# Block means of the first batch by products on TensorE, with a new order of the first jobs

## The chip, the cores and the metric

One core of a Trainium2 chip runs the whole program. The metric is the device time of one execution in microseconds; the median of three runs is used. The engines named below are PE (TensorE, matrix products), DVE (VectorE), ACT (ScalarE), POOL (GpSimd) and SP (SyncE, which here only issues DMAs).

## The reference

Attention over 2 batches of 8 heads, 768 tokens, head size 64: each query sees the keys within 15 tokens of it, and 24 summaries, one for each block of 32 tokens. The summary of the values is the block mean, `v_sum` below. Two MLPs with 512 to 2048 to 512 channels follow, over all 1536 tokens.

```python
k_sum = k.reshape(B, H, nb, block, D).max(axis=3)
v_sum = v.reshape(B, H, nb, block, D).mean(axis=3)
scores_l = scale * np.matmul(q, k.transpose(0, 1, 3, 2))
mask_l = np.abs(pos[:, None] - pos[None, :]) < window
scores_s = scale * np.einsum('bhsd,bhnd->bhsn', q, k_sum) + np.log(block)
a = softmax(concatenate([where(mask_l, scores_l, -1e9), scores_s]))   # in short
x = np.matmul(a, np.concatenate([v, v_sum], axis=2))                   # attention out
h = x @ w_in1;  x2 = (max(h, 0) + alpha * min(h, 0)) @ w_out1
h = x2 @ w_in2; out = (P(h) / (Q(h) + 1e-6)) @ w_out2                  # P cubic, Q quadratic
```

## The kernel before

**Jobs and stages.** The tokens are cut into four chunks of 384 (CH). An attention job is one pair of heads of one chunk: job j is pair j % 4 of chunk j // 4, 16 jobs in all. A job has the stages KQ (transposes of keys and queries on PE, copies by ACT, block maxima by DVE), KX (the rest of the keys, first chunk of a batch only), SC (scores on PE, mask and row minimum on DVE, exponential on ACT), NM (normalising on DVE), TR (transposes of the probabilities on PE, copied to `pt` by ACT) and PV (product with the values on PE, split into `x_hi` by ACT and `x_lo` by DVE). The value operand of a PV has 120 rows (KU): 96 rows of a window of values (KW) for each of six units of 64 queries, and below them the 24 block means, the same for each unit.

**The first chunk.** Jobs 0 to 3 run alone at the start, in orders written out by hand, one list an engine: FIRST_PE, FIRST_ACT, FIRST_DVE. WI and WO in FIRST_ACT are copies of a weight tile to `w_in_hi` or `w_out_hi`, each followed by a subtraction on POOL that makes the low part. RUN_UP puts products of the identity, read by nobody, ahead of a stage on PE, 26 in nine places. EARLY puts the first quarters of `hidden1(0)` and `hidden1(1)` between the last stages of jobs 2 and 3.

**The block means.** POOL makes them for four heads at once: `summarise_values(g)` adds 32 rows in a tree of five additions on 96 partitions, after a 768 KB load (`load_v_blocks`). For the first chunk `spread_first_sums` then writes them six times over into `vw0`, the values of jobs 0 to 3, by DMAs that POOL issues itself. `pt` is one buffer, so the copy of job j's probabilities waits for the PV of job j - 1 (`pe_v`).

**The loop of the first MLP.** STEPS = 64 steps, 16 a chunk. A step is `hidden1(i)` (12 products of 384 columns) and `output1(i - 2)` (12 more). Between them `slot(c + 1, f, n)` puts the stages of the next chunk's jobs, by the table SLOTS, and by SOON for the first job of the second chunk (job 4). `hidden1(i)` waits for `g1_low(i - 2)` on DVE, which waits for `g1_high(i - 2)` on ACT. In the first steps ACT also makes the high parts of the weights, in program order with everything else:

```python
if c == 0:
    for n in (f + 3,) if f < 2 else (2 * f + 1, 2 * f + 2) if f < 4 else (f + 5,):
        if n < FT:
            weights(0, n)
...
if i >= R1:
    act.wait_ge(pe_o, i - R1 + 1)
    g1_high(i)
```

so that tiles 5 and 6 come in step 2 ahead of `g1_high(2)`, and tiles 7 and 8 in step 3. Weight tiles are loaded by two: `load_w(0, 3)` brings tiles 6 and 7.

**The queue of loads.** SP issues all loads in one program order. `load_keys(5)` waits there for `pe_k` of job 4, that is, for the four key transposes of job 4 on PE, because both jobs use the same buffer. Behind it in the queue stand `load_values(4)` and `load_w(0, 3)`.

Of the kernel before, what the change touches and what calls it, by code (L numbers as in the profile page):

```python
# [13 lines left out]
def attention_two_mlps(nc, q, k, v, w_in1, w_out1, alpha, w_in2, w_out2, a_coef, b_coef, out):  # L14
# [32 lines left out]
    VG = 4  # L47
# [13 lines left out]
    KQ, KX, SC, NM, TR, PV, WI, WO = range(8)  # L61
# [5 lines left out]
    FIRST_PE = [(0, KQ), (0, KX), (1, KQ), (0, SC), (1, KX), (2, KQ), (0, TR), (1, SC), (2, KX), (3, KQ),  # L67
                (1, TR), (2, SC), (3, KX), (3, SC), (0, PV), (2, TR), (1, PV), (3, TR), (2, PV), (4, KQ), (3, PV)]

    FIRST_ACT = [(0, KQ), (1, KQ), (0, SC), (2, KQ), (0, TR), (1, SC), (3, KQ), (1, TR), (2, SC), (0, PV),  # L70
                 (3, SC), (0, WI), (2, TR), (1, PV), (1, WI), (3, TR), (2, PV), (4, KQ), (3, PV), (0, WO), (2, WI), (1, WO),
                 (2, WO)]

    FIRST_DVE = [(0, KQ), (0, KX), (1, KQ), (0, SC), (1, KX), (0, NM), (2, KQ), (1, SC), (2, KX), (1, NM), (3, KQ),
                 (2, SC), (3, KX), (2, NM), (3, SC), (0, PV), (3, NM), (1, PV), (2, PV), (4, KQ), (3, PV)]
# [24 lines left out]
    vs_raw1 = place("vs_raw1", [P, BLOCK * D], offset=w_end - (UNITS * H + BLOCK) * D * 4)  # L100
# [12 lines left out]
    vs_raw0 = place("vs_raw0", [P, BLOCK * D], offset=top)  # L113
# [6 lines left out]
    vs_raw = [vs_raw1 if g == 1 else vs_raw0 for g in range(VG)]  # L120
# [4 lines left out]
    kx_raw = place("kx_raw", [P, 4, 2, D])  # L125
    q_raw = place("q_raw", [P, QTILES, 2, D])
# [6 lines left out]
    pt = place("pt", [P, UNITS, P])  # L133
# [3 lines left out]
    g_neg = place("g_neg", [P, CH])  # L137
    g1_hi = place("g1_hi", [P, R1, CH], F32R)
# [15 lines left out]
    with ExitStack() as ctx:  # L154
# [19 lines left out]
        sums0_loaded = [sem(f"sums0_loaded{n}") for n in range(2)]  # L174
# [8 lines left out]
        pe_s, pe_t, pe_v = sem("pe_s"), sem("pe_t"), sem("pe_v")  # L183
# [26 lines left out]
        def batch(j):  # L210
            return chunk(j) // 2
# [11 lines left out]

        def kx_jobs(j):

            return sum(1 for n in range(j + 1) if half(n) == 0)
# [16 lines left out]
        def vgroup(j):  # L243
            return batch(j) * 2 + pair(j) // 2
# [12 lines left out]
        def _(sp):  # L257
# [5 lines left out]
            def load_first_keys(p):  # L263
                hs = heads(p)
                load_pair(k_raw0[:, :, hs, :], KROWS[0], k[0, hs, 0:4 * KROWS[0], :], k0_loaded[p])
                load_pair(q_raw0[:, :, hs, :], P, q[0, hs, 0:CH, :], q0_loaded[p])
                load_pair(kx_raw0[:, :, hs, :], KXROWS, k[0, hs, 4 * KROWS[0]:S, :], kx0_loaded[p])
# [30 lines left out]
            def load_first_edges():  # L298
# [4 lines left out]
            def load_first_windows(p):  # L303
                for h in range(2 * p, 2 * p + 2):
                    sp.dma_start(vw0[0:KW, 1:UNITS, h, :], windows_of(0, h, 0)).then_inc(v0_loaded[p], 16)

            def load_values(j):
                b, h0, s = batch(j), 2 * pair(j), j % 2
                if j >= NPAIR + 2:
                    sp.wait_ge(pe_v, j - 1)  # L310
                t0, t1 = (1, UNITS) if half(j) == 0 else (0, UNITS - 1)
                for h in range(2):
                    sp.dma_start(vw[0:KW, s, t0:t1, h, :], windows_of(b, h0 + h, half(j))).then_inc(v_loaded[s], 16)
                t, rows, inside, outside = edge(half(j))
                sp.dma_start(vw[rows, s, t, :, :], v[b, h0:h0 + 2, inside, :].rearrange("h p d -> p h d")).then_inc(v_loaded[s], 16)
                sp.dma_start(vw[outside, s, t, :, :], v[b, h0:h0 + 2, 0:WINDOW, :].rearrange("h p d -> p h d")).then_inc(v_loaded[s], 16)
                sp.wait_ge(pool_vs, vgroup(j) + 1)
                for h in range(2):
                    r = (pair(j) % 2) * 2 * NB + h * NB
                    src = vsum[r:r + NB, vgroup(j), :].unsqueeze(1).broadcast_to([NB, UNITS, D])  # L320
                    sp.dma_start(vw[KW:KU, s, :, h, :], src).then_inc(v_loaded[s], 16)

            def load_v_blocks(g):
                if g >= 2:
                    sp.wait_ge(pool_vs, 2 * g - 3)
                sp.dma_start(vs_raw[g][0:4 * NB, :],
                             v[g // 2, 4 * (g % 2):4 * (g % 2) + 4].rearrange("h (n j) d -> (h n) (j d)", j=BLOCK)).then_inc(vs_loaded[g], 16)
# [26 lines left out]
            load_first_edges()  # L354
            load_first_windows(0)
            load_first_windows(1)
# [4 lines left out]
            load_w_out(0, 0)  # L361
            load_w(0, 1)
# [12 lines left out]
            load_v_blocks(2)  # L375
            load_values(6)
            load_keys(7)
            load_v_blocks(3)
# [16 lines left out]
        def _(pool):  # L395
# [23 lines left out]

            tree = 0  # L420

            def summarise_values(g):

                nonlocal tree
                pool.wait_ge(vs_loaded[g], 16)
                n = BLOCK * D // 2
                while n >= D:
                    rows = vs_raw[g][0:4 * NB]
# [4 lines left out]
                pool.tensor_scalar(vsum[0:4 * NB, g, :], vs_raw[g][0:4 * NB, 0:D], 1.0 / BLOCK, 1.0,  # L433
                                   ALU.mult, ALU.mult).then_inc(pool_vs, 1)

            def spread_first_sums(g):

                pool.wait_ge(pool_vs, g + 1)
                for h in range(4):
                    pool.dma_start(vw0[KW:KU, :, 4 * g + h, :],  # L440
                                   vsum[h * NB:(h + 1) * NB, g, :].unsqueeze(1).broadcast_to([NB, UNITS, D])).then_inc(sums0_loaded[g], 16)
# [12 lines left out]
            for g in range(2):  # L454
                summarise_values(g)
                spread_first_sums(g)
            for f in range(WG):
                split_w_in(f)
            for f in range(FT):
                if f >= WG:  # L460
                    split_w_in(f)
                split_w_out(0, f)
                if f in (11, 15):
                    summarise_values(2 + f // 15)
# [16 lines left out]
        def _(act):  # L481
# [3 lines left out]
            def attention(j, stage):  # L485
# [30 lines left out]
                elif stage == TR:  # L516
                    for h in range(2):
                        act.wait_ge(pe_t, 2 * j + h + 1)
                        if j and h == 0:
                            act.wait_ge(pe_v, j)  # L520
                        copy(pt[0:KU, h * UP:(h + 1) * UP, :].rearrange("p n c -> p (n c)"), bk[h][0:KU, 0:UP * P]).then_inc(act_pt, 1)
# [13 lines left out]

# [266 lines left out]
        def _(pe):  # L802
            def attention(j, stage):
# [12 lines left out]
                if stage == KQ:  # L816
# [8 lines left out]
                    if first:  # L825
                        pe.wait_ge(q0_loaded[p], 32)
                    else:
# [20 lines left out]
                elif stage == TR:  # L848
                    for g in range(2):
# [3 lines left out]
                        last.then_inc(pe_t, 1)  # L853
                elif stage == PV:
                    if first:
                        pe.wait_ge(edges0_loaded, 32)
                        pe.wait_ge(v0_loaded[p], 32)
                        pe.wait_ge(sums0_loaded[p // 2], 16 * 4)
# [3 lines left out]
                    for u in range(UNITS):  # L862
                        for h in range(2):
                            rows, tokens = slice(h * QT, (h + 1) * QT), slice((u % 2) * QT, (u % 2 + 1) * QT)
                            values = vw0[0:KU, u, 2 * p + h, :] if first else vw[0:KU, s, u, h, :]
                            last = pe.matmul(bk[0][rows, u * QT:(u + 1) * QT], values, pt[0:KU, h * UP + u // 2, tokens],  # L866
# [91 lines left out]

            pe.wait_ge(pool_ready, 1)
            for j, stage in FIRST_PE:  # L960
                spare = acc[3] if FIRST_PE.index((j, stage)) < FIRST_PE.index((3, KQ)) else att[1]
                for _ in range(RUN_UP.get((j, stage), 0)):
                    pe.matmul(spare[:, 0:P], ident[:, :], ident[:, :], start=True, stop=True)
                attention(j, stage)
                for i, pairs in EARLY.get((j, stage), []):
                    hidden1(i, pairs)
# [3 lines left out]
            for i in range(STEPS):  # L970
                c, f = i // FT, i % FT
                begun = [kk for parts in EARLY.values() for n, pairs in parts for kk in pairs if n == i]
                hidden1(i, range(len(begun), KD))
# [43 lines left out]
```

## Time and profile before

| what | value |
|---|---|
| median of 3 runs | 632.59 us (632.51 to 634.97) |
| profiled execution, its own time | 633.66 us |
| its span, first to last instruction | 631.8 us |
| PE busy | 613.3 us, 97% of the span |
| weight loads into PE | 571.4 us, 90% |
| DVE, ACT, POOL busy | 413.6, 309.0, 201.5 us |
| PE in the chain that ended last | 92% |
| bytes moved by DMA | 37.60 MB |

A busy share is a mean over stages of different kinds. The share of a stretch, and what ends the idle time in it, is read from the windows, the timelines and the chain. All times are microseconds from the start of the span.

### The profile page before, as it was taken

Reading aid. Unit: us, or ns where it says so; the run is one execution under the profiler, and the core shown is the slowest. Engines: PE = TensorE matmul, PEld = TensorE weight load, DVE = VectorE, ACT = ScalarE, POOL = GpSimd, SP = SyncE. Lnnn points to the kernel's source line nnn. Section 1 sums busy time; section 2 is a strip of 40 time slices with the busy share of each in tenths; the row PEclk is TensorE's granted clock in tenths of the full one; section 3 lists DMA queues with packets and bytes.
Section 4 is the critical chain, followed back from the end, with each engine's and each line's share of the span. In section 5 each row is a group of like instructions: output and inputs, shape, how many; then the busy total and the mean of one; then the engine's idle time right before and its main releaser. Section 6 shows DMA issues by size and latency. Waiting matters only on the chain.

```text
span 631.8 us, 10645 instructions
## 1 busy us (share of the span) xinstructions
PE 613.3 (97%) x3941; PEld 571.4 (90%) x3941; DVE 413.6 (65%) x953; ACT 309.0 (49%) x774; POOL 201.5 (32%) x224
## 2 busy tenths in 40 slices
PE   7588999999999999999999999999999999999998
PEld 7478999999999999999999989899989998999996
DVE  4445554566456544555555499878887888788775
ACT  4267544342232423232234477656765666556654
POOL 2839676000000000000133366334443444334431
PEclk9688999999999999999999999999999999999999
DMA  8978862022201221001433300001000000001001
GB/s 181 211 201 240 220 124 49 14 63 61 57 15 42 50 50 40 11 2 34 125 110 106 127 34 1 1 0 52 1 0 2 23 29 1 0 2 51 0 2 50
DMA packets 79187, 37.60 MB, mean 60 GB/s; under 512 B 56624, under 2 KB 73024, under 8 KB 78752
## 3 DMA queue, kind: packets, MB, share of 16 engines
q1 hardware_dynamic: 78880, 36.63, 22.8%
q8 instruction: 31, 0.51, 0.3%
q0 software_dynamic: 256, 0.30, 0.2%
q14 instruction: 20, 0.16, 0.1%
HBM read 32.58 MB, written 3.15 MB: 57 GB/s over the span
## 4 chain that ended last, share of the span: by engine, by line
PE 92%; DVE 2%; DMA 2%; SPq 1%; POOL 1%; ACT 1%; issue 0%; ACTq 0%; DVEq 0%; POOLq 0%
PE acc L876 15%; PE acc L878 14%; PE acc L877 14%; PE hid L876 11%; PE hid L878 10%; PE hid L877 10%; PE att L876 4%; PE att L878 4%; PE att L877 4%; PE att L866 2%; PE att L812 2%; PE att L845 1%; SPq L261 1%; PE att L852 1%; DMA vs_raw<-in_v_dram 1%; POOL vs_raw L429 1%
## 5 line engine op out<-in xcount | busy, mean ns | idle before, releaser
L876 PE MATMUL hid<-x_hi,w_in_hi 128*128 128x384 f32 x384 | 130.9, 341 | 2.6 <-DVE g_lo L725 1.8
L878 PE MATMUL hid<-x_hi,w_in_lo 128*128 128x384 f32 x384 | 129.8, 338 | 0.0
L877 PE MATMUL hid<-x_lo,w_in_hi 128*128 128x384 f32 x384 | 129.5, 337 | 0.0
L451 POOL TENSOR_TENSOR w_out_lo<-w_out_raw,w_out_hi 128x512 fp32r<-128x512 f32 x32 | 41.3, 1292 | 239.8 <-ACT w_out_hi L483 239.8
L876 PE MATMUL acc<-g_hi,w_out_hi 128*128 128x384 f32 x256 | 91.2, 356 | 0.0
L473 POOL TENSOR_SCALAR qpart<-habs,ab 128x384 f32<-128x384 f32 x64 | 44.0, 688 | 143.1 <-ACT poly L627 142.4
L878 PE MATMUL acc<-g_hi,w_out_lo 128*128 128x384 f32 x256 | 86.8, 339 | 0.0
L877 PE MATMUL acc<-g_lo,w_out_hi 128*128 128x384 f32 x256 | 86.5, 338 | 0.0
L483 ACT ACTIVATE g_hi<-hid 128x384 fp32r<-128x384 f32 x96 | 48.4, 504 | 71.1 <-PE acc L878 63.7
L725 DVE TENSOR_TENSOR g_lo<-hid,g_hi 128x384 fp32r<-128x384 f32 x64 | 35.6, 556 | 66.3 <-ACT g_hi L483 66.3
L876 PEld LDWEIGHTS hid<-x_hi,w_in_hi 128*128 128x128 f32 x384 | 72.5, 189 | 4.9 <-POOL w_in_lo L446 2.1
L878 PE MATMUL acc<-w_out_hi,g_lo 128*128 128x512 f32 x192 | 76.1, 396 | 0.0
L877 PE MATMUL acc<-w_out_lo,g_hi 128*128 128x512 f32 x192 | 75.6, 394 | 0.0
L876 PE MATMUL acc<-w_out_hi,g_hi 128*128 128x512 f32 x192 | 75.5, 393 | 0.0
L877 PEld LDWEIGHTS hid<-x_lo,w_in_hi 128*128 128x128 f32 x384 | 72.6, 189 | 1.3
L878 PEld LDWEIGHTS hid<-x_hi,w_in_lo 128*128 128x128 f32 x384 | 72.5, 189 | 0.0
L748 DVE TENSOR_SCALAR g_neg<-hid,prelu_alpha 128x384 f32<-128x384 f32 x64 | 39.4, 616 | 48.9 <-PE hid L878 48.9
L475 POOL TENSOR_TENSOR qpart<-qpart,habs 128x384 f32<-128x384 f32 x64 | 65.7, 1026 | 5.3
L876 PEld LDWEIGHTS acc<-g_hi,w_out_hi 128*128 128x128 f32 x256 | 48.2, 188 | 2.6 <-issue 1.7
L877 PEld LDWEIGHTS acc<-g_lo,w_out_hi 128*128 128x128 f32 x256 | 48.3, 189 | 0.0
L878 PEld LDWEIGHTS acc<-g_hi,w_out_lo 128*128 128x128 f32 x256 | 48.1, 188 | 0.0
L513 ACT ACTIVATE att<-att,nmax 128x120 f32<-128x120 f32 x78 | 24.7, 368 | 44.4 <-DVE nmax L693 44.4
(145 smaller groups left out, 1159.6 us busy)
## 6 DMA issues: line engine op xcount, KB each, us to landing
w_in_raw<-in_moe_w_in_dram SPq DMA_DIRECT2D x32, 256.0 KB, 4.2
w_out_raw<-in_moe_w_out_dram SPq DMA_DIRECT2D x16, 512.0 KB, 4.2
vw<-in_v_dram SPq DMA_DIRECT2D x32, 120.0 KB, 5.3
q_raw<-in_q_dram SPq DMA_DIRECT2D x32, 96.0 KB, 2.6
vs_raw<-in_v_dram SPq DMA_DIRECT2D x4, 768.0 KB, 7.0
out_dram<-out_sb SPq DMA_DIRECT2D x12, 256.0 KB, 2.0
k_raw<-in_k_dram SPq DMA_DIRECT2D x16, 104.0 KB
k_raw<-in_k_dram SPq DMA_DIRECT2D x16, 100.0 KB
```

Source lines behind the costliest of these rows:

```text
L451: pool.tensor_tensor(w_out_lo[:, f, :], w_out_raw[:, f, :], w_out_hi[f][:, :].bitcast(F32), ALU.subtract).then_inc(pool_w_out, 1)
L473: pool.tensor_scalar(qpart[:, i % 2, :], habs[:, i % 2, :], ab[:, 5:6], ab[:, 4:5], ALU.mult, ALU.add).then_inc(pool_qb, 1)
L475: pool.tensor_tensor(qpart[:, i % 2, :], qpart[:, i % 2, :], habs[:, i % 2, :], ALU.mult).then_inc(pool_q, 1)
L483: return act.activation(dst, src, ACT.Identity)
L513: last = act.activation(scores_of(bk, h, n), scores_of(bk, h, n), ACT.Exp, scale=-1.0, bias=nmax[:, s, i:i + 1], accum_out=sums_of(bk, h)[ ...
L725: dve.tensor_tensor(g1_lo[:, i % R1, :], hid[i % 2][:, 0:CH], g1_hi[:, i % R1, :].bitcast(F32), ALU.subtract).then_inc(dve_g, 1)
L748: dve.tensor_scalar(g_neg[:, :], hb, 0.0, prelu_alpha[:, f:f + 1], ALU.min, ALU.mult).then_inc(dve_m, 1)
L812: tr = pe.transpose(dst[:, t * rows:(t + 1) * rows], rows_of_pair.rearrange("p h d -> p (h d)"), ident[0:rows, 0:rows])
L866: last = pe.matmul(bk[0][rows, u * QT:(u + 1) * QT], values, pt[0:KU, h * UP + u // 2, tokens], start=True, stop=True)
L876: pe.matmul(dst, lhs[0], rhs[0], start=start, stop=False)
L877: pe.matmul(dst, lhs[0], rhs[1], start=False, stop=False)
L878: return pe.matmul(dst, lhs[1], rhs[0], start=False, stop=stop)
```

## The change

The block means of batch 0 are made on PE: a stage AV of ten accumulating products for each job multiplies six windows of values, and four tiles of the rest of the sequence (`v_rest`), by shifted columns of a matrix `avg` that holds 1/32 at the rows of a block. The means of a pair arrive in rows 96 to 119 of a PSUM bank, where ACT (stage SU) copies them six times over into `vw0`. POOL's tree stays for batch 1; a copy on POOL keeps the means of batch 0 for chunk 1 (`keep_first_sums`). `pt` has two buffers. The three lists are new; the early quarters of `hidden1` stand in FIRST_PE as HD, all eight; job 4's KQ moves from the lists to the loop (step 0), its SC to step 2. Weight subtractions on POOL run in another order. The first loads are issued in another order. The identity's products are 19 in five places.

```diff
-    SOON = {(0, 1): [SC], (1, 1): [NM], (2, 1): [TR], (3, 0): [PV]}
+    SOON = {(0, 2): [KQ], (2, 0): [SC], (2, 2): [NM], (3, 0): [TR], (3, 2): [PV]}
+    FIRST_PE = [(0, KQ), (0, KX), (1, KQ), (0, SC), (1, KX), (2, KQ), (1, SC), (0, AV), (0, TR), (2, KX), (3, KQ),
+                (2, SC), (1, AV), (1, TR), (3, KX), (0, PV), (2, AV), (3, SC), (2, TR), (3, AV), (1, PV), (2, PV),
+                (3, TR), (0, HD), (3, PV), (0, HD), (0, HD), (1, HD), (0, HD), (1, HD), (1, HD), (1, HD)]
+    RUN_UP = {(0, KQ): 8, (0, KX): 3, (0, SC): 3, (1, SC): 2, (2, KX): 3}
+    FIRST_ACT = [(0, KQ), (1, KQ), (0, SC), (2, KQ), (0, SU), (0, TR), (1, SC), (3, KQ), (1, SU), (1, TR), (2, SC),
+                 (2, SU), (0, PV), (2, TR), (3, SC), (0, WI), (1, PV), (3, SU), (3, TR), (1, WI), (2, PV), (3, PV),
+                 (2, WI), (0, WO), (1, WO), (2, WO)]
-    RUN_UP = {(0, KQ): 8, (0, KX): 2, (1, KQ): 1, (0, SC): 2, (0, TR): 4, (2, TR): 3, (1, PV): 2, (3, TR): 2, (2, PV): 2}
-    EARLY = {(3, TR): [(0, (0, 1))], (2, PV): [(1, (0, 1))], (3, PV): [(0, (2,)), (1, (2,))]}
...
-    pt = place("pt", [P, UNITS, P])
+    pt = place("pt", [P, 2, UNITS, P])
...
+            def first_rest(p):
+                hs = heads(p)
+                sp.dma_start(v_rest[0:RP, hs, :], v[0, hs, CH:S, :].rearrange("h (p t) d -> p h (t d)", t=RT)).then_inc(rest0_loaded[p], 16)
...
-            load_first_keys(0)
-            load_first_keys(1)
-            load_first_keys(2)
-            load_v_blocks(0)
-            load_first_keys(3)
-            load_v_blocks(1)
+            first_k(0)
+            first_q(0)
+            first_kx(0)
+            first_k(1)
+            first_q(1)
+            first_kx(1)
+            first_rest(0)
+            first_k(2)
+            first_q(2)
+            first_edges()
+            first_windows(0)
+            first_k(3)
+            first_q(3)
+            first_kx(2)
+            first_rest(1)
+            first_windows(1)
+            first_kx(3)
+            first_windows(2)
+            first_rest(2)
...
             load_w_in(0, 0)
-            load_first_windows(2)
-            load_first_windows(3)
-            load_keys(4)
+            first_windows(3)
+            first_rest(3)
             load_w_out(0, 0)
-            load_w(0, 1)
+            load_w_in(0, 1)
+            load_keys(4)
+            load_w_out(0, 1)
...
+            own = avg[0:KW, KW + 2 * (UNITS - 1):KW + 2 * UNITS]
+            own_rest = avg[0:RP, AW + KW + CH // BLOCK:AW + KU]
+            pool.memset(avg[:, :], 0.0).then_inc(pool_avg, 1)
...
+            def keep_first_sums():
+
+                pool.wait_ge(act_su, NPAIR)
+                pool.wait_ge(pool_w_in, WG)
+                pool.tensor_copy(vsum0.rearrange("p a h d -> p (a h d)"),
+                                 vw0[KW:KU, 0, :, :].rearrange("p h d -> p (h d)")).then_inc(pool_v0, 1)
+                pool.wait_ge(pool_v0, 1)
...
-            for g in range(2):
-                summarise_values(g)
-                spread_first_sums(g)
-            for f in range(WG):
-                split_w_in(f)
+            split_w_in(0)
+            split_w_in(1)
+            keep_first_sums()
+            split_w_in(2)
             for f in range(FT):
-                if f >= WG:
-                    split_w_in(f)
                 split_w_out(0, f)
+                if f + 3 < FT:
+                    split_w_in(f + 3)
...
-                        if j and h == 0:
-                            act.wait_ge(pe_v, j)
+                        if j >= 2 and h == 0:
+                            act.wait_ge(pe_v, j - 1)
...
+                elif stage == SU:
+                    act.wait_ge(pe_av, j + 1)
+                    copy(vw0[KW:KU, :, heads(p), :].rearrange("p u h d -> p u (h d)"),
+                         means_of(j)[KW:KU, :].unsqueeze(1).broadcast_to([NB, UNITS, P])).then_inc(act_su, 1)
...
+                elif stage == AV:
+                    if j == 0:
+                        pe.wait_ge(pool_avg, 5)
+                        pe.wait_ge(edges0_loaded, 32)
+                    pe.wait_ge(v0_loaded[p], 32)
+                    pe.wait_ge(rest0_loaded[p], 16)
+                    if j == 1:
+                        pe.wait_ge(act_pt, 2)
+                    if j:
+                        pe.wait_ge(act_su, j)
+                    means = means_of(j)[0:KU, :]
+                    for u in range(UNITS):
+                        at = 2 * (UNITS - 1 - u)
+                        pe.matmul(means, avg[0:KW, at:at + KU], vw0[0:KW, u, heads(p), :].rearrange("p h d -> p (h d)"),
+                                  start=u == 0, stop=False)
+                    for t in range(RT):
+                        last = pe.matmul(means, avg[0:RP, AW:AW + KU], v_rest[0:RP, heads(p), t * D:(t + 1) * D],
+                                         start=False, stop=t == RT - 1)
```

## Rows read from the trace of the kernel before

**Rows 1.** Windows: us, busy us and count per engine, PEclk, DMA share, GB/s.

```profile
16.00:29.30 13.30, 6.49 (x76) 4.47 (x70) 6.73 (x37) 2.96 (x15) 12.32 (x14) 0.68 1.14 217
...
62.70:631.80 569.10, 564.60 (x3496) 529.69 (x3495) 383.76 (x829) 275.85 (x663) 163.90 (x175) 1.00 0.16 43
```

**Rows 2.** Chain that ended last: start us, us, what.

```profile
9.63 6.24 DMA vs_raw<-in_v_dram
...
24.08 4.96 DMA vw<-vsum
...
29.32 1.57 PE att L866 x24
```

**Rows 3.** Timeline of POOL: start, us, line, op, tiles, count [idle <-releaser].

```profile
1.20 0.29 POOL L398 TENSOR_SCALAR_AFFINE_SELECT ident<-ident 128x128 f32<-128x128 f32 x1 [0.25 <-POOL ident L396]
...
16.02 5.42 POOL L429 TENSOR_TENSOR vs_raw<-vs_raw 96x1024 f32<-96x1024 f32 x5 [10.22 <-DMA vs_raw<-in_v_dram]
...
38.03 1.27 POOL L446 TENSOR_TENSOR w_in_lo<-w_in_raw,w_in_hi 128x512 fp32r<-128x512 f32 x1 [4.85 <-ACT w_in_hi L483]
```

**Rows 4.** Timeline of PE, same columns.

```profile
12.22 1.06 PE L963 MATMUL acc<-ident 128*128 128x128 f32 x8
...
38.40 0.82 PE L852 MATMUL acc<-ident,probs 128*120 128x128 f32 x6
...
41.64 0.92 PE L866 MATMUL acc<-pt,vw 120*64 120x64 f32 x24
42.49 0.44 PE L876 MATMUL hid<-x_hi,w_in_hi 128*128 128x384 f32 x1
...
43.12 0.33 PE L876 MATMUL hid<-x_hi,w_in_hi 128*128 128x384 f32 x1
...
43.89 0.56 PE L812 MATMUL att<-ident,k_raw 100*128 100x100 f32 x4
...
44.72 0.92 PE L866 MATMUL acc<-pt,vw 120*64 120x64 f32 x24
...
47.54 0.85 PE L845 MATMUL att<-kt,qt 64*64 64x120 f32 x24
...
50.94 0.41 PE L876 MATMUL hid<-x_hi,w_in_hi 128*128 128x384 f32 x1 [1.84 <-DVE g_lo L725]
...
62.70 0.34 PE L876 MATMUL hid<-x_hi,w_in_hi 128*128 128x384 f32 x1
...
64.81 0.51 PE L812 MATMUL att<-ident,k_raw 100*128 100x100 f32 x4
```

**Rows 5.** Windows of two us, columns as in the first group.

```profile
20.00:22.00 2.00, 1.70 (x28) 1.41 (x27) 0.76 (x2) 0.01 (x1) 1.52 (x4) 0.67 1.21 174
36.00:38.00 2.00, 2.00 (x28) 1.69 (x27) 1.86 (x9) 1.95 (x11) 0.00 (x0) 0.56 1.06 257
52.00:54.00 2.00, 2.00 (x8) 2.00 (x7) 1.88 (x6) 2.00 (x5) 1.72 (x2) 0.50 0.85 250
```

**Rows 6.** Timeline of SP's DMA issues.

```profile
44.49 0.79 SPq L261 DMA_DIRECT2D k_raw<-in_k_dram  x2
...
51.01 1.07 SPq L334 DMA_DIRECT2D w_in_raw<-in_moe_w_in_dram  x2
52.13 0.51 SPq L341 DMA_DIRECT2D w_out_raw<-in_moe_w_out_dram  x1
```

**Rows 7.** DMA issues at 18.4, 51.0, 52.1 us: KB each, us to landing.

```profile
vw<-in_v_dram SPq DMA_DIRECT2D x2, 120.0 KB, 5.7
...
w_in_raw<-in_moe_w_in_dram SPq DMA_DIRECT2D x2, 256.0 KB, 3.1
...
w_out_raw<-in_moe_w_out_dram SPq DMA_DIRECT2D x1, 512.0 KB, 5.5
```

**Rows 8.** Timeline of ACT.

```profile
56.26 0.88 ACT L483 ACTIVATE pt<-att 120x384 f32<-120x384 f32 x2 [2.12 <-PE att L852]
...
58.58 0.63 ACT L483 ACTIVATE w_out_hi<-w_out_raw 128x512 fp32r<-128x512 f32 x1
```

More of the change, by code:

```diff
@@ L46, in attention_two_mlps @@
     QTILES = CH // P
-    VG = 4
+    VG = 2
+    RT = 4
+    RP = (S - CH) // RT
     STEPS = NCH * FT
@@ L112, in attention_two_mlps @@
     x_lo = place("x_lo", [P, 2, KD, CH], F32R)
-    vs_raw0 = place("vs_raw0", [P, BLOCK * D], offset=top)
+    vs_raw = place("vs_raw", [P, BLOCK * D], offset=top)
+    v_rest = place("v_rest", [P, H, RT * D], offset=top)
     y_raw = place("y_raw", [P, 2, KD, CH])
@@ L137, in attention_two_mlps @@
     g_neg = place("g_neg", [P, CH])
+    AW = KU + 2 * (UNITS - 1)
+    avg = place("avg", [P, AW + KU], offset=top - CH * 4)
     g1_hi = place("g1_hi", [P, R1, CH], F32R)
@@ L173, in attention_two_mlps @@
         edges0_loaded = sem("edges0_loaded")
-        sums0_loaded = [sem(f"sums0_loaded{n}") for n in range(2)]
+        rest0_loaded = [sem(f"rest0_loaded{p}") for p in range(NPAIR)]
         k_loaded, kx_loaded, q_loaded = sem("k_loaded"), sem("kx_loaded"), sem("q_loaded")
@@ L243, in vgroup @@
         def vgroup(j):
-            return batch(j) * 2 + pair(j) // 2
+            return pair(j) // 2
         def banks(j):
@@ L427, in summarise_values @@
                 while n >= D:
-                    rows = vs_raw[g][0:4 * NB]
+                    rows = vs_raw[0:4 * NB]
                     pool.tensor_tensor(rows[:, 0:n], rows[:, 0:n], rows[:, n:2 * n], ALU.add).then_inc(pool_tree, 1)
@@ L432, in summarise_values @@
                     n //= 2
-                pool.tensor_scalar(vsum[0:4 * NB, g, :], vs_raw[g][0:4 * NB, 0:D], 1.0 / BLOCK, 1.0,
+                pool.tensor_scalar(vsum[0:4 * NB, g, :], vs_raw[0:4 * NB, 0:D], 1.0 / BLOCK, 1.0,
                                    ALU.mult, ALU.mult).then_inc(pool_vs, 1)
[L436 to L441, printed above, removed]
+            def keep_first_sums():
[4 more added lines that the diff above has]
+                pool.wait_ge(pool_v0, 1)
             def split_w_in(f):
@@ L534, in w_in_high @@
                 act.wait_ge(w_in_loaded[f // WG], 16 * WG * (m + 1))
+                if m == 0 and f == 3:
+                    act.wait_ge(pool_v0, 1)
                 copy(w_in_hi[f][:, :, :].rearrange("p k c -> p (k c)"), w_in_raw[:, f, :, :].rearrange("p k c -> p (k c)")).then_inc(act_w_in, 1)
@@ L865, in attention @@
                             values = vw0[0:KU, u, 2 * p + h, :] if first else vw[0:KU, s, u, h, :]
-                            last = pe.matmul(bk[0][rows, u * QT:(u + 1) * QT], values, pt[0:KU, h * UP + u // 2, tokens],
+                            last = pe.matmul(bk[0][rows, u * QT:(u + 1) * QT], values, pt[0:KU, s, h * UP + u // 2, tokens],
                                              start=True, stop=True)
@@ L957, in output2 @@
                         mm.then_inc(pe_y, 1)
+            begun = [0, 0]
             pe.wait_ge(pool_ready, 1)
             for j, stage in FIRST_PE:
-                spare = acc[3] if FIRST_PE.index((j, stage)) < FIRST_PE.index((3, KQ)) else att[1]
                 for _ in range(RUN_UP.get((j, stage), 0)):
[L963 to L966, printed above, removed]
+                    pe.matmul(acc[2][:, 0:P], ident[:, :], ident[:, :], start=True, stop=True)
+                if stage == HD:
+                    hidden1(j, [begun[j]])
+                    begun[j] += 1
+                else:
+                    attention(j, stage)
                 if (j, stage) == (2, PV):
@@ L971, in _ @@
                 c, f = i // FT, i % FT
-                begun = [kk for parts in EARLY.values() for n, pairs in parts for kk in pairs if n == i]
-                hidden1(i, range(len(begun), KD))
+                if i >= 2:
+                    hidden1(i)
                 slot(c + 1, f, 0)
```

76 lines of the change are left out of this document (48 added, 28 removed).

## The prediction

> **What bounds the kernel now.** I read the windows of the whole span first, to see where PE is not busy. From 62.7 us to the end it works 564.6 of 569.1 us at full granted clock [rows 1]. No instruction of that stretch is taken away, so there is nothing to win there, and the page's 97% for PE says the same. What is open lies before 62.7. From 16.0 to 29.3 PE works 6.49 of 13.30 us [rows 1]. The chain that ended last says why: a 768 KB load of value blocks (6.24 us from 9.63), POOL's tree, the DMA of the means into the values (4.96 us from 24.08), and only then the first PV at 29.32 [rows 2]. POOL's own timeline adds that it sat idle for 10.22 us before the tree, and that the five additions took 5.42 us [rows 3]. In this thin stretch the granted clock fell (mean 0.67 in 20 to 22 us) and it was still at its lower level, 1.2 GHz, for most of 36 to 38 us (mean 0.56) [rows 5]. So the beginning is bound by one chain through DMA and POOL. A second place is at 50.94, where PE waited 1.84 us for `g_lo` [rows 4] and the clock fell again (0.50 in 52 to 54) [rows 5].
>
> **The place where both kernels are compared.** I compare the start of `hidden1(4)`, at 62.70 before [rows 4]. By then both programs have done the same products of the MLP (steps 0 to 3, outputs 0 and 1) and all of job 4. Behind it the order on PE is the same, so whatever this point gains is the gain of the run, if no later stall is new.
>
> **Part 1: the block means leave the chain.** AV needs the windows of values, `v_rest` and `avg`. The two fills and four selects that make `avg` are bounded below by nothing and above by 0.29 us each, the select over 128 columns [rows 3]: under 2 us, on a POOL that is idle until 16.02 [rows 3]. Cost: nothing, and about 1 us if POOL were late. The values of pair 0 are in the queue behind 2176 KB in all (two pairs of keys and queries with their rest 1152, `v_rest` 192, k2 and q2 400, edges 192, windows 240). At 217 GB/s, that is 212 KB a us [rows 1], it takes 10.3 us, and with the first issue at 0.75 us and some 3 us until a queue that is still being filled is in full flow I take 14.8 us as the landing (13.5 to 17.0: the late end is an issue at 11.3 plus the 5.7 us that a window took to land [rows 7]). So the first AV starts at about 14.8, where the old chain gave 29.3 to the first PV.
>
> **Part 2: what PE does from there.** It is now the engine with the longest queue. Four products of the identity, 8 instructions, take 1.06 us with a last one of 0.25, so one instruction is 0.115 us [rows 4]. An AV is ten such products, 20 instructions: 2.3 us. No row shows these; the bounds are 0.09 and 0.18 us an instruction (1.8 to 3.6 us for an AV), the upper one if weights of 120 shifted columns cannot be loaded beside the products. I take 2.3 since the products of the identity have the same shape. In the order of FIRST_PE, from the start of the first AV to the end of job 4's key transposes:
> - four AV: 9.2 us;
> - four TR at 0.60 (six transposes, 0.82 busy with 0.2 of tail): 2.4;
> - three products of the identity: 0.7;
> - two KX at 0.40 and KQ of job 3 at 0.83 (43.89 to 44.72): 1.6;
> - two SC at 0.78 (0.85 busy): 1.6;
> - four PV at 0.85 (41.64 to 42.49): 3.4;
> - eight quarters of `hidden1` at 0.60 (0.63 from 42.49 to 43.12): 4.8;
> - the transpose of alpha 0.2, and four key transposes 0.5.
> All from [rows 4]; the sum is 24.4. ACT and DVE have less: ACT 4.9 us for each job (KQ 1.1, exponentials 1.8, SU 0.8, `pt` 0.9, `x_hi` 0.4), DVE some 5. SU is a copy of 768 columns; `pt` takes 0.44 for 384 and a weight tile of 512 columns 0.52 to its successor [rows 8], so 0.8, bounds 0.5 and 1.1. In my order of the stages on the three engines PE then waits only some tenths for `x_lo` and for a scale of the probabilities; I add 0.4. Job 4's key transposes end at 14.8 + 24.4 + 0.4 = 39.6 us, before at 44.45 (43.89 and 0.56) [rows 4]. That is 4.85 us earlier. The second buffer of `pt` is what lets TR run ahead of PV; its cost is nothing. The copy of the means on POOL (bounds 0.3 and 1.3, the subtraction of 512 columns [rows 3]) stands ahead of the third weight subtraction, which is done at about 38.3 and needed at 40: hidden; uncovered it would cost up to 1.3.
>
> **Part 3: what comes late next.** KQ of job 4 now stands directly ahead of `hidden1(2)`, where it was 50.94 - 44.72 = 6.2 us ahead [rows 4]. SP waits for it before it issues anything more: the keys of job 5 went out at 44.49, `w_in` 6 and 7 at 51.01 and `w_out` 6 and 7 at 52.13 [rows 6]. The latter landed 5.5 us later, at 57.6 [rows 7]. The same queue, moved by 4.85, lands it at 52.8. ACT wants it in step 2, ahead of `g1_high(2)`, at about 46.5, and it is in program order: `g1_high(2)`, both copies of job 4's `pt` and everything after them stand behind the wait. Copy of tile 6 0.5, `g_hi` 0.4, two `pt` 0.88 [rows 8], PV of job 4 0.85 [rows 4]: `hidden1(4)` starts at 52.8 + 2.65 = 55.45. PE alone would be there sooner: from 40.0 it has two `hidden1` and two `output1` of 2.11 (62.70 to 64.81 [rows 4]), SC 0.78, TR 0.6 and PV 0.85, to 50.7. So PE stands still for 4.8 us. Before, an idle time of 1.84 was enough to bring the clock down soon after; I expect that here too. PV at the low clock is 1.57 [rows 2] instead of 0.92 [rows 4]: 0.65; and the products that follow cost up to twice for a while. For both I take 1.8, bounds 0 and 3: the low stretch before was about 3.5 us long, which at half rate loses 1.75. `hidden1(4)` counts as started at 57.2, so the gain is 62.7 - 57.2 = 5.5 us.
>
> **Part 4: what costs nothing.** Seven products of the identity fewer: they stood in idle time. The loads: 1536 KB of blocks go, 768 KB of `v_rest` come, and 288 KB of means on POOL's queue go, so the first weight tiles come earlier (I have `w_in` 0 at about 25, wanted at 31). POOL's new order of subtractions puts the tree of batch 1 about three steps of ACT later; its means are wanted a chunk later. If that cover were gone, a wait of up to 5.4 us (the tree [rows 3]) could stand at the change of chunk.
>
> **The sum.** Span 631.8 - 5.5 = 626.3. The profiled execution took 633.66, 1.86 more than its span and 1.07 above the median of 632.59; against its own time the sum gives 628.2, against the median 627.1. I forecast 627.1. Its own range is 624.5 to 629.5 (AV 1.8 to 3.6 us each is the widest term, and then the clock).
>
> **Rivals.**
> - *Weights are no wait.* If ACT is not held up by tiles 6 and 7, `hidden1(4)` starts at 50.7 to 51.0 and the gain is 11.7: 620.9. Against it: SP's seven microseconds of issues ahead of those tiles [rows 6] are the same ones. For it: fewer bytes are in flight then. 10%.
> - *The first values come late.* If windows land at 17.0 rather than 14.8, PE idles over 3 us after the second SC, with a stretch of transposes before it. 2.2 us are lost, and the clock may fall, which costs another 2: a gain of 1.3, 631.3. For it: window DMAs took 5.7 us [rows 7] and they stand behind ten other issues. 18%.
> - *Slower: the clock stays low through the first jobs.* Before, it was low for some 16 us, from about 21 to 38 [rows 5], with short blocks and waits between them. If it falls ahead of the first AV and does not come back until the quarters of `hidden1`, each block costs about 1.75 times as much (PV 1.57 for 0.92). Over 20 us of low clock that loses 20 x (1 - 1/1.75) = 8.6 us, and the result is 635.7. It decides against the change from about 13 us of low clock. Against it: AV is 2.3 us of dense products, four times, with hardly a gap. 8%.
> - *The means are not what held PV.* Then the first PV would still come at 29; but the chain of waits names the DMA of the means directly. Near 632.6; 4%.
>
> On the third rival the Trainium skill speaks against this change. "TensorE: Matmul & The Clock Gate", section "HAM oscillation — how this bites in real kernels", says that bursts of products with waits for data between them each begin at half clock. By that rule every AV that waits for its values would run at 1.2 GHz, four times 2.3 more, and the sum would be some 9 us later, an estimate. The trace agrees for the wait at 50.94, and for the thin stretch from 16 us on.
>
> **How the numbers follow.** Forecast 60%, the rivals 10, 18, 8 and 4%. The range has to leave out no more than 2 in 10: it takes the forecast's own range, the late values (to 632) and the larger part of the first rival: 621.5 to 632.0. About 0.5%, 3.2 us, is what a measurement can tell from no change, so faster means below 629.4. The forecast lies there nearly whole (57 of 60), the first rival too, and of the late values a third: 0.73. Slower than 635.8: 0.07. Within: 0.20.
>
> **What would show it.** The first AV at 14 to 15.5 us and 2.3 us long; no DMA from `vsum` and no tree on POOL in the first 60 us; key transposes of job 4 near 39 us; then a wait of 3 to 6 us on PE before PV of job 4 or `hidden1(4)`, ended by ACT's `pt` or `g_lo`, with ACT idle until a copy of `w_out_raw`; a low clock behind it; `hidden1(4)` at 55 to 57; from there the same 569 us. The prediction is wrong if AV takes 3.6 us, if the clock is low between 15 and 38 us, or if the tiles 6 and 7 land before ACT wants them.

## The result and the profile after

The changed kernel takes 627.15 us, the median of four runs (626.75 to 628.32), against 633.04 for the kernel before: ratio 0.990, interval 0.9881 to 0.9918. On another chip later it was 628.00 against 634.53, 0.9902 (0.9883 to 0.9921). The forecast was 627.1. The span of the profiled execution went from 631.8 to 626.6 us; that execution of the changed kernel, at 628.32 us, is the slowest of its four, so spans show 5.2 us of gain where the medians show 5.9.

The windows of the changed kernel, columns as in [rows 1]:

```profile
16.00:29.30 13.30, 12.60 (x163) 11.54 (x162) 8.62 (x44) 9.81 (x37) 0.00 (x0) 1.00 0.97 235
...
62.70:626.60 563.90, 559.39 (x3464) 524.52 (x3462) 382.45 (x825) 272.52 (x656) 160.97 (x172) 1.00 0.16 42
```

From 16 to 29.3 us PE is busy for 12.60 us where it was 6.49, and the granted clock is full where its mean was 0.68 [rows 1]. POOL, with 12.32 us of tree and DMA issues in that stretch before, does nothing there. Behind 62.7 us nothing was won.

The timeline of PE in the changed kernel (start, us, line, op, out<-in, count, and in brackets the idle time before and what ended it):

```profile
11.76 0.58 PE L869 MATMUL acc<-ident,k_raw 104*128 104x104 f32 x4 [1.50 <-DMA k_raw<-in_k_dram]
...
13.88 0.85 PE L904 MATMUL hid<-kt,qt 64*64 64x120 f32 x24
14.88 1.54 PE L926 MATMUL acc<-vw,avg 96*120 96x128 f32 x12
...
17.13 0.82 PE L911 MATMUL att<-ident,probs 128*120 128x128 f32 x6
...
29.56 1.54 PE L926 MATMUL att<-vw,avg 96*120 96x128 f32 x12 [0.51 <-issue]
...
39.89 0.51 PE L869 MATMUL att<-ident,k_raw 100*128 100x100 f32 x4
...
41.08 0.41 PE L954 MATMUL hid<-x_hi,w_in_hi 128*128 128x384 f32 x1 [0.35 <-DVE g_lo L782]
...
51.03 0.33 PE L956 MATMUL acc<-g_hi,w_out_lo 128*128 128x384 f32 x1
55.07 1.11 PE L944 MATMUL att<-pt,vw 120*64 120x64 f32 x24 [3.71 <-ACT pt L535]
56.12 0.69 PE L954 MATMUL hid<-x_hi,w_in_hi 128*128 128x384 f32 x1
...
59.64 0.51 PE L869 MATMUL att<-ident,k_raw 100*128 100x100 f32 x4
```

The first AV starts at 14.88 and takes 2.25 us (to 17.13). Job 4's key transposes end at 40.40 (39.89 and 0.51), before at 44.45 [rows 4]. Then the new wait: PE is through with `output1(1)` at 51.4 and stands still for 3.71 us until ACT has copied the probabilities of job 4 to `pt`. The keys of job 5, which come directly behind `hidden1(4)`, start at 59.64, before at 64.81 [rows 4]. That is 5.17 us earlier, and the span is 5.2 us shorter: all of the gain is made by this point. What stands behind the wait is shown by the queues of SP and ACT:

```profile
40.43 0.79 SPq L269 DMA_DIRECT2D k_raw<-in_k_dram  x2
...
47.26 0.51 SPq L365 DMA_DIRECT2D w_out_raw<-in_moe_w_out_dram  x1
```

```profile
50.05 0.63 ACT L535 ACTIVATE w_in_hi<-w_in_raw 128x512 fp32r<-128x512 f32 x1 [1.59 <-DMA w_in_raw<-in_moe_w_in_dram]
53.16 0.63 ACT L535 ACTIVATE w_out_hi<-w_out_raw 128x512 fp32r<-128x512 f32 x1 [2.48 <-DMA w_out_raw<-in_moe_w_out_dram]
...
54.07 0.86 ACT L535 ACTIVATE pt<-att 120x384 f32<-120x384 f32 x2
```

SP issues nothing from 32.4 us to 40.43, when job 4's key transposes are done, and comes to `w_out` of tiles 6 and 7 at 47.26. ACT waits 1.59 us for `w_in` and 2.48 us for `w_out` of tile 6, and `g_hi` and both copies of `pt` come after them. The chain of the changed kernel that ended last goes the same way:

```profile
47.26 5.88 DMA w_out_raw<-in_moe_w_out_dram
...
55.07 1.11 PE att L944 x24
```

The clock fell behind that wait, not in it. Windows of two us, with PEclk third from the end:

```profile
52.00:54.00 2.00, 0.00 (x0) 0.00 (x0) 0.00 (x0) 0.84 (x2) 1.25 (x2) 1.00 1.08 325
54.00:56.00 2.00, 0.93 (x24) 0.95 (x24) 1.65 (x3) 0.93 (x3) 0.00 (x0) 0.91 1.07 351
56.00:58.00 2.00, 2.00 (x10) 1.89 (x7) 0.56 (x1) 1.78 (x4) 0.69 (x1) 0.50 1.13 324
58.00:60.00 2.00, 2.00 (x13) 1.96 (x12) 0.72 (x2) 1.17 (x3) 2.00 (x3) 0.74 0.99 180
```

The mean of 0.91 comes from its end: the clock is still full from 55.2 to 55.6, half a microsecond into the PV, and at its lower level, 1.2 GHz, right after. So more than half of the PV ran at the full clock (1.11 us, between the 0.92 and 1.55 of a PV at either level) and most of `hidden1(4)` at the lower one.

### The profile page after: what moved, and what is told of

The parts are those of the page before. It is cut to its first block, busy times and chain, and to the rows that moved or that the text cites. A ratio compares the mean times of both kernels' runs of the same rounds, so it can differ in the third digit from the quotient of the medians.

```text
span 626.6 us, 10782 instructions
## 1 busy us (share of the span) xinstructions
PE 612.4 (98%) x4007; PEld 573.3 (92%) x4007; DVE 415.6 (66%) x953; ACT 311.8 (50%) x778; POOL 187.6 (30%) x212
## 4 chain that ended last, share of the span: by engine, by line
PE 93%; SPq 2%; DMA 2%; DVE 1%; ACT 1%; issue 1%; ACTq 0%
PE acc L954 15%; PE acc L956 14%; PE acc L955 14%; PE hid L954 10%; PE hid L955 10%; PE hid L956 10%; PE att L954 4%; PE att L956 4%; PE att L955 4%; PE att L944 2%; PE att L869 1%; PE att L904 1%; SPq L269 1%; PE att L911 1%; DMA w_out_raw<-in_moe_w_out_dram 1%; PE att L926 1%
```

## The experiments

Eleven variants were run, and the changed kernel once more. Each ratio is to the kernel before on the same chip, with its 95% interval. The changed kernel stands at 0.9901 (mean of its two). 0.001 is 0.63 us.

### The wait for weights: two ways round it

Edit of `w3_ahead`:

```diff
             load_w(0, 2)
+            load_w(0, 3)
             load_keys(5)
             load_values(4)
-            load_w(0, 3)
```

> The changed kernel with the loads of weight tiles 6 and 7 issued ahead of the keys of job 5, so that they no longer stand behind the wait for job 4's key transposes. Theory (in the changed kernel ACT's copies of job 4's probabilities stand behind the copy of w_out tile 6, which lands 12.8 us after those transposes): PE's wait of 3.7 us before the PV of job 4 goes, the granted clock stays at its upper level, hidden1(4) is as fast as its neighbours; what is left is up to 1 us of waiting for the values of job 4, which are issued 1.6 us later. 4.3 to 5.3 us below the changed kernel's 627.15, so 622 to 623. Rival (the wait has another cause that comes at nearly the same time, such as the values of job 4 or POOL's subtractions): under 1.5 us gained, 625.7 or more.

Measured: 622.33 us, 0.9813 (0.9795 to 0.9831): 5.6 us below the changed kernel. Its PE timeline:

```profile
38.23 0.51 PE L869 MATMUL att<-ident,k_raw 100*128 100x100 f32 x4
...
49.63 0.92 PE L944 MATMUL att<-pt,vw 120*64 120x64 f32 x24
...
52.69 0.51 PE L869 MATMUL att<-ident,k_raw 100*128 100x100 f32 x4
```

PV of job 4 has no wait. From job 4's keys to job 5's it is 14.46 us (52.69 less 38.23), in the changed kernel 19.75 (59.64 less 39.89). So 5.3 us are the price of the stall with its low clock, and the values of job 4, issued later, were still in time. The clock stays full to the end (mean 1.0). Its profiled execution is 6.9 us shorter than the changed kernel's, more than the 5.6 us of the ratios, because its first loads also happened to land earlier: the first AV starts at 13.98, 0.9 us before the changed kernel's, and job 4's keys at 38.23, 1.7 us before.

Edit of `tile6_later`, on ACT, with the loads untouched:

```diff
-                    for n in (f + 3,) if f < 2 else (2 * f + 1, 2 * f + 2) if f < 4 else (f + 5,):
+                    for n in (f + 3,) if f < 3 else (6, 7, 8) if f == 3 else (f + 5,):
```

> The changed kernel with the copies of weight tile 6 moved on ACT from step 2 to step 3, behind g1_high(2) and the probabilities of job 4; the loads are as they were. If the order on ACT passes the late load on to PE, PV of job 4 starts at about 51.5 us without a wait, and only g1_high(3) is late: a stall of 0 to 1.5 us at hidden1(5). 3.5 to 5.3 us below 627.15. If the late tiles are needed by PE itself at that time, or ACT is late for another reason, nothing is gained (626.5 to 627.5).

Measured: 623.31 us, 0.9826 (0.9806 to 0.9846), 4.8 us below the changed kernel. The timeline of ACT:

```profile
48.09 0.87 ACT L535 ACTIVATE pt<-att 120x384 f32<-120x384 f32 x2
...
54.78 0.63 ACT L535 ACTIVATE w_out_hi<-w_out_raw 128x512 fp32r<-128x512 f32 x1 [0.30 <-DMA w_out_raw<-in_moe_w_out_dram]
```

`pt` is copied at 48.09, six us earlier than in the changed kernel, and no wait appears on PE. The loads are as late as they were, so it was the order on ACT that handed a late load to PE; the tiles themselves were not needed yet. Either change removes the stall, and the two agree.

### What held the first jobs before: means and buffer

Three versions of the kernel before. `before_pt2` has the second buffer of `pt`, with `act.wait_ge(pe_v, j - 1)` for j of 2 and more, and nothing else. `before_no_means` leaves out the block means of the first chunk and puts zeros in their rows. With them go POOL's four DMAs for each group of heads (288 KB in all) and the wait for them; the trees on POOL stay:

```diff
+            pool.memset(vw0[KW:KU, :, :, :], 0.0).then_inc(sums0_loaded[0], 1)
             tree = 0
...
-                spread_first_sums(g)
...
-                        pe.wait_ge(sums0_loaded[p // 2], 16 * 4)
+                        pe.wait_ge(sums0_loaded[0], 1)
```

> The kernel before with two buffers of transposed probabilities and nothing else of the change. Theory (the means' chain is the wall and the single buffer only passes it on): the probabilities of jobs 1 to 3 are ready before the means arrive, the PVs of jobs 0 and 1 follow at 29 to 31 us, and PV of job 2 waits for the second set of means at about 38 us, before 41.6: 2 to 3.5 us faster than before. Rival (the single buffer is the larger half of the loss): 5 us or more. Rival (the buffer is not on the path): under 0.5.

Measured: 630.99 us, 0.9951 (0.9935 to 0.9968), 3.1 us faster.

> The kernel before with the block means of the first chunk left out (zeros in their rows; the trees on POOL stay for the second chunk, the DMAs that spread them and the wait for them go). One buffer of probabilities as before. Theory: the first PV starts when the windows of pair 0 have landed and the scores of job 3 are done, at about 25 instead of 29.3 us, and everything behind it moves with it: 3 to 4.5 us faster than before. If something else bounds the first PV: under 1 us.

Measured: 630.64 us, 0.9939 (0.9916 to 0.9961), 3.9 us faster by the ratio.

> The kernel before with both: two buffers of probabilities and no block means in the first chunk. Theory: means and buffer together are the whole wall, so this gains more than the two alone together, 6 to 11 us against before, limited by the landing of windows (31 us) and weights; the step list then meets the wait for weight tiles 6 and 7. If the two gains only add up: 5 to 7 us.

Measured: 625.62 us, 0.9872 (0.9850 to 0.9894), 8.1 us faster. The same places in the three timelines of PE, the first PV and job 4's keys:

```profile
30.99 1.55 PE L866 MATMUL att<-pt,vw 120*64 120x64 f32 x24 [5.60 <-DMA vw<-vsum]
...
39.81 0.92 PE L866 MATMUL acc<-pt,vw 120*64 120x64 f32 x24
...
42.06 0.56 PE L812 MATMUL att<-ident,k_raw 100*128 100x100 f32 x4
```

```profile
26.56 1.55 PE L866 MATMUL att<-pt,vw 120*64 120x64 f32 x24 [1.42 <-issue]
...
41.15 0.56 PE L812 MATMUL att<-ident,k_raw 100*128 100x100 f32 x4
```

```profile
26.20 1.55 PE L866 MATMUL att<-pt,vw 120*64 120x64 f32 x24
...
36.43 0.56 PE L812 MATMUL att<-ident,k_raw 100*128 100x100 f32 x4
...
43.48 0.41 PE L876 MATMUL hid<-x_hi,w_in_hi 128*128 128x384 f32 x1 [1.84 <-DVE g_lo L725]
```

With the buffer alone PE waits 5.60 us for the DMA of the means, and PV of job 2 comes at 39.81, before at 41.64 [rows 4]. With the means alone gone the first PV comes at 26.56, before at 29.32 [rows 2], but the next copies of `pt` still queue behind the PVs, as ACT's timeline of that run shows:

```profile
28.21 0.87 ACT L483 ACTIVATE pt<-hid 120x384 f32<-120x384 f32 x2 [8.66 <-PE att L866]
```

Together job 4's keys start at 36.43: 7.5 us earlier than before, against 1.8 and 2.7 for each alone. In these executions the two are worth more together than apart, though part of that is chance: the execution of `before_pt2` is the slowest of its six, and its first PV, at 30.99, came 1.7 us later than before. From job 4's keys to job 5's it is 20.9 us in the kernel before and with either change alone, and 20.0 with both, where the clock stayed up. The times do not settle it: 1.28% for both against 1.10% for the sum, which is inside the intervals. That each of the two is on the path, and that both together are worth 8.1 us, is shown.

### The buffer in the new order

`after_pt1` is the changed kernel with the old rule for `pt`: slot 0 always, and a wait for the PV before.

> The changed kernel with one buffer of transposed probabilities, and each copy of them waiting for the PV before, as in the kernel before; all else as changed. Theory: ACT's copies for jobs 1 to 3 wait for the PVs of jobs 0 to 2, and with them the exponentials of jobs 2 and 3; job 4's key transposes end 3 to 4 us later and so does everything: 2.5 to 4.5 us slower than 627.15, around 630.5. If the second buffer is not needed in this order: within 1 us of 627.15.

Measured: 634.00 us, 1.0002 (0.9986 to 1.0017). The whole gain is gone, 6.4 us and not 2.5 to 4.5. The two timelines, ACT and PE:

```profile
33.31 0.87 ACT L535 ACTIVATE pt<-acc 120x384 f32<-120x384 f32 x2 [3.37 <-PE hid L944]
```

```profile
43.48 0.51 PE L869 MATMUL att<-ident,k_raw 100*128 100x100 f32 x4
...
59.62 1.55 PE L944 MATMUL att<-pt,vw 120*64 120x64 f32 x24 [4.65 <-ACT pt L535]
...
64.98 0.51 PE L869 MATMUL att<-ident,k_raw 100*128 100x100 f32 x4
```

The mechanism is the expected one: ACT stands 3.37 us for a PV, and job 4's keys come at 43.48, 3.6 us later. What was mis-sized is what follows: the wait on PE behind it is 4.65 instead of 3.71 us, the PV runs wholly at the low clock (1.55 us), and job 5's keys are 5.3 us later than in the changed kernel (64.98 against 59.64). So the buffer is no detail: in this order it is worth as much as the whole change.

### How much of the start is PE's own work

`short_av` leaves out the four products with `v_rest` in each AV (the means of the later blocks of batch 0 are then missing).

> The changed kernel with the four products of the rest of the sequence left out of each AV (the block means of the later part of batch 0 are then wrong): 8 instructions of about 0.11 us less, four times, 3.6 us of PE's work between 15 and 33 us. If PE alone bounds the first jobs, as the prediction's sum took it: 3.2 to 3.6 us faster than 627.15. If ACT, DVE and the loads stand close behind PE: 1 to 2 us faster. If the loads bound it: under 0.5.

Measured: 624.71 us, 0.9864 (0.9825 to 0.9903); three of its four runs lie between 624.46 and 624.73. By the ratio it is 2.3 us faster than the changed kernel at 0.9901, which its interval just includes, and by the medians 3.4. In its profile job 4's keys start at 36.65, 3.2 us earlier, of which 0.7 came with an earlier first AV (14.16). That leaves 2.5 of the 3.6 us removed. One row of its PE timeline, and the landing of `v_rest` of pair 3, issued at 21.87, show where 0.9 of the rest went:

```profile
27.22 1.54 PE L926 MATMUL att<-vw,avg 96*120 96x128 f32 x12 [0.89 <-issue]
```

```profile
v_rest<-in_v_dram SPq DMA_DIRECT2D x1, 192.0 KB, 5.3
```

21.87 and 5.3 us give 27.2, where the last AV starts. The answer lies between the two expectations: in this profile PE bounds most of the stretch, and the loads, rather than ACT or DVE, stand about 1 us behind it.

### The products of the identity

`few_run_up` keeps only the first eight: `RUN_UP = {(0, KQ): 8}`.

> The changed kernel without the products of the identity but the first eight: 11 of 19 are left out. If they only fill time: 0.4 to 1.0 us faster than 627.15 (three of them stand on the path after the first AV, 0.65 us, the others in waits for loads). If they hold the clock: the granted clock falls before or in the first AV, the AVs of jobs 0 and 1 take up to 4.5 us instead of 2.3, and the run is 2 to 5 us slower than 627.15.

Measured: 628.01 us, 0.9895 (0.9878 to 0.9912), no difference from the changed kernel. But the profile is not the same:

```profile
13.99 2.88 PE L926 MATMUL acc<-vw,avg 96*120 96x128 f32 x12 [0.44 <-DMA vw<-in_v_dram]
...
18.37 1.49 PE L911 MATMUL att<-ident,probs 128*120 128x128 f32 x6
...
40.65 0.51 PE L869 MATMUL att<-ident,k_raw 100*128 100x100 f32 x4
...
54.87 1.55 PE L944 MATMUL att<-pt,vw 120*64 120x64 f32 x24 [2.75 <-ACT pt L535]
```

The clock was at 0.50 from 14 to 20 us, the first AV took 4.38 us (13.99 to 18.37) instead of 2.25, and still job 4's keys were only 0.8 us later. The longer AV, the transposes behind it and the next keys cost 3.1 us. Against that, this execution's first AV had started 0.9 us earlier, the three products on the path (0.67 us) were gone, and behind the scores of job 2 another 0.8 us went, the pause at 29.56 among it; the other eight products had stood in waits. Then PE's wait for the weights came out at 2.75 instead of 3.71 us and took the rest in, although the whole PV behind it ran at the low clock. So I took the stall away and tried again. `w3_few_run_up` and `w3_no_kx2` both have the loads of `w3_ahead`; the second drops only the three products ahead of job 2's KX.

> The loads of tiles 6 and 7 ahead, as in w3_ahead, and only the first eight products of the identity. In few_run_up the clock was at 1.2 GHz from 13.9 to 20.3 us and the step list was 0.8 us late at job 4's keys, while the wait for weights behind it was 1 us shorter. Without that wait nothing can give the time back. If the eleven products pay for themselves by the clock: 0.5 to 1.5 us slower than w3_ahead (0.9813 of before), 0.982 to 0.984. If not: equal or faster.

> The loads of tiles 6 and 7 ahead, as in w3_ahead, and the three products of the identity ahead of job 2's KX left out (16 stay). They stand behind ten dense products of an AV and ahead of transposes, a score stage and the next AV. If the clock holds without them: 0.3 to 0.7 us faster than w3_ahead, 0.980 to 0.981 of before. If it falls between 18 and 20 us: 1 to 2 us slower than w3_ahead.

Measured on one chip: 624.46 us, 0.9841 (0.9821 to 0.9862), runs from 623.01 to 624.78, and 621.78 us, 0.9802 (0.9784 to 0.9820), runs from 621.08 to 622.11. The eight products by which they differ are worth 2.7 us once nothing behind hides it. Against `w3_ahead`, on another chip, all eleven are worth 1.8 us by the ratios, a little over the expected 0.5 to 1.5. In `w3_no_kx2` the clock stayed full; its gain over `w3_ahead` (0.9802 against 0.9813) is inside the intervals. Its timeline says why little was to be had:

```profile
18.16 0.49 PE L869 MATMUL acc<-ident,kx_raw 88*128 88x88 f32 x4 [0.97 <-DMA kx_raw<-in_k_dram]
```

The place of the three products is taken by a wait of 0.97 us for the rest of job 2's keys.

### The first values, later

`late_windows` issues `first_edges` and `first_windows(0)` behind `first_k(3)`, `first_q(3)` and `first_kx(2)`.

> The changed kernel with the edges and windows of pair 0 issued behind the keys and queries of job 3 and the rest of job 2's keys: 576 KB are put ahead of them, at 200 KB a us some 2.9 us. If the first values bound the first AV (the prediction's second rival): the first AV starts at 16.8 to 18 instead of 14 to 14.9, PE stands still for 3 us ahead of it, job 4's key transposes end 2.5 to 3 us later with the clock up, 4.5 to 5 us later if it falls; the run is 2.5 to 5 us slower than the changed kernel. If there is slack between the loads and PE: under 1 us.

Measured: 632.48 us, 0.9972 (0.9959 to 0.9985), 4.4 us slower than `after_again`, the changed kernel on the same chip.

> The changed kernel as it is, to have it on the chip of the three below: 626.5 to 628.3 us, ratio to before 0.99.

```profile
17.52 2.83 PE L926 MATMUL acc<-vw,avg 96*120 96x128 f32 x12 [3.79 <-DMA vw<-in_v_dram]
...
21.85 1.49 PE L911 MATMUL att<-ident,probs 128*120 128x128 f32 x6
...
26.81 1.57 PE L926 MATMUL att<-vw,avg 96*120 96x128 f32 x12
...
29.09 0.82 PE L911 MATMUL hid<-ident,probs 128*120 128x128 f32 x6
...
45.10 0.51 PE L869 MATMUL att<-ident,k_raw 100*128 100x100 f32 x4
```

PE waits 3.79 us, the first AV starts at 17.52 and takes 4.33 us at the low clock. The second is at the full one again (2.28 us from 26.81). Job 4's keys are 5.2 us later than in the changed kernel's first profile and 6.2 later than in that of `after_again` (38.86). The execution shown, at 634.58 us, is the slowest of its ten, so the 4.4 us of the medians are the measure of the loss and the places of the timeline overstate it. This is the prediction's second rival, made to happen: it had put the loss at 4.2 us.

## Why the prediction came out right

| step | forecast | measured |
|---|---|---|
| first AV starts, its length | 14.8, 2.3 us | 14.88, 2.25 us |
| job 4's key transposes end | 39.6 | 40.40 |
| `w_out` of tiles 6 and 7 lands | 52.8 | 53.1 (47.26 and 5.88) |
| PE's wait ahead of PV of job 4 | 4.8 us | 3.71 us |
| `hidden1(4)` starts | 55.45 | 56.12 |
| lost to the low clock, PV and `hidden1(4)` | 1.8 us | 1.6 us |
| gain, span | 5.5 us | 5.2 us |

**The bound and the place of comparison** held: PE is busy for 559.4 of 563.9 us behind 62.7, and the gain is complete at the keys of job 5. There was no wait at the change of chunk.

**Part 1 and 2.** The start of the first AV, 14.88 for 14.8, came out closer than its reasoning, by luck. The terms given for the landing, 10.3 us of transfer, 0.75 and some 3, add up to 14.05 and not to 14.8. And in this execution it was not the values that set the start. The two DMAs of pair 0's windows, issued from 10.24 to 11.21, landed after:

```profile
vw<-in_v_dram SPq DMA_DIRECT2D x2, 120.0 KB, 3.5
```

That gives about 14.3 us, while PE, held up for 1.50 us by job 2's keys at 11.76, was in the scores of job 1 until 14.7. In `after_again`, the same kernel, the keys came sooner and the AV did wait for its values:

```profile
14.23 1.54 PE L926 MATMUL acc<-vw,avg 96*120 96x128 f32 x12 [0.48 <-DMA vw<-in_v_dram]
```

The price of an AV, taken from the products of the identity, was right to 2%. From the first AV to the end of job 4's key transposes it took 25.5 us, where the sum and its 0.4 us for waits gave 24.8. Of the waits 0.51 is the pause ahead of job 3's AV at 29.56, where the profile names no releaser. The landing of `v_rest` of pair 3, issued at 22.32, is:

```profile
v_rest<-in_v_dram SPq DMA_DIRECT2D x1, 192.0 KB, 7.2
```

22.32 and 7.2 us give 29.5, and the AV's program asks for this load: it waited for it. I had looked at the landing of pair 0 alone and allowed 0.4 us for all waits; another 0.46 us went at the scores of job 2, behind DVE's maxima, and 0.22 at job 3's PV. The copy of the means on POOL was hidden.

**Part 3** carries the prediction. Without the wait for weights I would have said 620.9 (the first rival), and `w3_ahead` and `tile6_later` are that case: 622.33 and 623.31, 5.6 and 4.8 us below the changed kernel, where the rival's distance was 6.2. The stall was 1.1 us shorter than forecast because PE came to it later by 1.5 us (51.4, where the forecast's sum has 50.7 less the 0.85 of the PV), while ACT set the PV free later by only 0.5 (55.07 for 54.6), the load having landed 0.3 later. Of the 1.5, 0.8 come from the lateness of the key transposes and 0.35 from a wait of `hidden1(2)` for `g_lo` (41.08), for which the sum had nothing. Since the load and not PE set the PV's start, the span came out within 0.3 us. The agreement of 627.15 with 627.1 is closer than that, and luck has a part in it: the forecast took 5.5 us off 632.59, and measured were 5.9 off 633.04.

**Part 4** weighed the products of the identity by idle time alone. No run tests the seven that were taken away. Of those that stay most do stand in waits, yet eight of them are worth 2.7 us by the clock.

**The part of the second buffer.** I gave its cost as nothing and its use in one sentence. `after_pt1` shows 6.4 us. A reader of the prediction would have put the gain down to the means alone; `before_no_means` shows 3.9 us for that.

**The rivals.** Late values cost 4.4 us when made to happen. The first rival's 620.9 lies outside the range that was said to take in its larger part. The rival of the low clock did not come, and the rule beside it, that bursts with waits between them each begin at half clock ("TensorE: Matmul & The Clock Gate", section "HAM oscillation — how this bites in real kernels", of the Trainium skill), was applied too widely: in the changed kernel no AV waited for more than 0.51 us and all four ran at the full clock, and even in `late_windows` only the one behind the long wait ran low. Its point that a burst behind a wait for data runs low agrees with what followed the 3.79 us there and the 3.71 us ahead of the PV of job 4; but the second burst began at the full clock, which fell half a microsecond into it.

## What to carry to other kernels

When work is brought forward, look for the loads whose issue hangs on it: here one wait in SP's program order (the keys of job 5) tied a load of weights to an instruction that now stood just ahead of its use, and one line moved gave nearly as much again (0.990 to 0.981). A late load reaches the bounding engine through whichever in-order engine meets it first, so the copy that waits for it belongs behind the copies that are due sooner (here 4.8 us). And a stall hides other costs: the products of the identity looked worthless until the stall behind them was gone.

## What the runs showed of the hardware beyond what I expected

The length of a wait alone did not say whether the clock falls. At the same place and with the same wait (1.83 or 1.84 us) ahead of `hidden1(2)`, the clock fell in the kernel before [rows 5], in `before_pt2` and in `before_no_means`, and stayed up in `before_pt2_no_means`. Its windows:

```profile
42.00:44.00 2.00, 0.52 (x3) 0.55 (x4) 1.97 (x11) 1.76 (x12) 2.00 (x2) 1.00 0.95 195
44.00:46.00 2.00, 2.00 (x13) 2.00 (x12) 1.86 (x7) 2.00 (x7) 1.48 (x2) 1.00 0.30 53
```

And in `few_run_up` it fell at about 13.9 us, behind transposes and scores with no wait over 0.5 us from 8 us on, with PE busy for 1.20 and 1.26 us of the two windows from 10 to 14. In the changed kernel's first profile PE was busy for 0.50 and 1.37 us of the same two windows and the clock stayed up, so the busy time of that stretch alone does not tell the two apart. No run tells which part of the work before is the reason.

Nor does the fall have to come while PE stands still. Ahead of the PV of job 4 it came half a microsecond after the end of a wait of 3.71 us in the changed kernel, about 0.1 us before the end of one of 3.95 us in `after_again`, and right at the end of one of 2.75 us in `few_run_up`. So the same block was paid at 1.11, 1.55 and 1.55 us.

Prices of the same block at the lower and at the full clock: an AV 4.38 us (`few_run_up`) and 2.25, a PV of 24 instructions 1.55 (`after_pt1`) and 0.92 (`w3_ahead`).
